# Attention ahead of a mixture of experts: the order of q, k and V loads, the form of two masks, minima per tile, and the place of one copy

## The reference, cut to what matters

```python
batch, n_heads, seq, head_dim = (2, 8, 768, 64);  n_sink, window = (4, 128)
scores = scale * np.matmul(q, k.transpose(0, 1, 3, 2))
keep = is_sink | in_window            # is_sink: key < 4; in_window: 0 <= query - key < 128
scores = np.where(keep, scores, -1000000000.0)
a = np.exp(scores - np.max(scores, axis=-1, keepdims=True))
a = a / (np.sum(a, axis=-1, keepdims=True) + 1e-09)
attn_out = np.matmul(a, v)
```

## Time and profile before

| what | us |
|---|---|
| timed executions | 810.29, 810.45, 813.3; median 810.45 |
| profiled execution | 813.45 |
| its span, first to last instruction | 811.7 |
| PE busy in the span | 768.5 |
| DVE, ACT, POOL busy | 508.9, 285.6, 314.4 |
| first scores / last value matmuls of the attention | 7.0 / 127.7 |

### The profile page before, as it was taken

How to read it: one execution, slowest core, us unless ns; L and a number is a source line. 1 busy time by engine, 2 the same in 40 slices (tenths; PEclk the granted TensorE clock), 3 DMA queues, 4 the chain that set the end, 5 groups by cost and what they waited for, 6 DMA issues and landing times.

```text
span 811.7 us, 13212 instructions
## 1 busy us (share of the span) xinstructions
PE 768.5 (95%) x4198; PEld 631.6 (78%) x4199; DVE 508.9 (63%) x874; ACT 285.6 (35%) x594; POOL 314.4 (39%) x331
## 2 busy tenths in 40 slices
PE   8878794899999999999999999998999999999997
PEld 4666673788888888888888888886888888888886
DVE  5555686444545545445445445457998888888776
ACT  6665571303030300303012300045554555544453
POOL 5367782846473370925618372660111011000000
PEclk9988997799999999999999999999999999999999
DMA  5445565453544270632616272220100110001001
GB/s 162 152 132 147 174 183 195 155 170 117 170 163 135 73 224 26 200 110 90 194 39 224 86 229 73 74 65 0 53 27 26 52 27 27 0 14 40 0 1 52
DMA packets 49485, 82.85 MB, mean 102 GB/s; under 512 B 18080, under 2 KB 22240, under 8 KB 49440
## 3 DMA queue, kind: packets, MB, share of 16 engines
q1 hardware_dynamic: 31440, 33.89, 12.8%
q10 hardware_dynamic: 13600, 33.96, 12.7%
q0 software_dynamic: 4400, 14.42, 6.4%
HBM read 66.01 MB, written 16.25 MB: 101 GB/s over the span
## 4 chain that ended last, share of the span: by engine, by line
PE 84%; DVE 6%; ACT 3%; DMA 3%; issue 3%; SPq 1%; POOL 0%; ACTq 0%; DVEq 0%; POOLq 0%
PE bank L1297 21%; PE bank L1308 21%; PE bank L1369 15%; PE bank L1350 15%; PE bank L1281 3%; DMA k_in<-in_k 2%; PE bank L1202 2%; PE bank L1274 2%; PE bank L1177 2%; ACT probs L657 2%; PE bank L1186 1%; PE bank L1211 1%; DVE bank L834 1%; PE bank L1161 1%; PE bank L1342 0%
## 5 line engine op out<-in xcount | busy, mean ns | idle before, releaser
L562 POOL TENSOR_TENSOR wgt<-stage,wgt 128x1024 f32 (+1 forms) x64 | 151.2, 2401 | 108.9 <-ACT wgt L720 108.9
L1308 PE MATMUL bank<-wgt,hT 128*128 (+1 forms) x744 | 186.1, 399 | 0.0
L1297 PE MATMUL bank<-wgt,xT 128*128 (+1 forms) x744 | 183.9, 396 | 1.5 <-DVE xT L1043 1.5
L1297 PEld LDWEIGHTS bank<-wgt,xT 128*128 128x128 f32 x744 | 138.4, 189 | 29.4 <-DVE xT L1043 1.7
L720 ACT ACTIVATE wgt<-stage 128x1024 f32 (+1 forms) x64 | 61.6, 1045 | 271.3 <-PE bank L1308 261.2
L1308 PEld LDWEIGHTS bank<-wgt,hT 128*128 128x128 f32 x744 | 135.1, 188 | 25.9
L1369 PE MATMUL bank<-wgt,gT 128*128 128x512 f32 x576 | 141.3, 395 | 4.8 <-DVE gT L1104 4.8
L1350 PE MATMUL bank<-x2T,wgt 128*128 128x512 f32 (+1 forms) x588 | 138.2, 385 | 0.9 <-DVE x2T L1081 0.9
L1369 PEld LDWEIGHTS bank<-wgt,gT 128*128 128x128 f32 x576 | 108.5, 190 | 28.6 <-DVE gT L1104 6.1
L1350 PEld LDWEIGHTS bank<-x2T,wgt 128*128 128x128 f32 x588 | 108.7, 188 | 23.0 <-POOL wgt L634 1.1
L1049 DVE TENSOR_SCALAR h<-bank 128x512 f32<-128x512 f32 x62 | 42.9, 691 | 66.7 <-PE bank L1297 66.7
(11 more groups left out here) (166 smaller groups left out, 955.9 us busy)
## 6 DMA issues: line engine op xcount, KB each, us to landing
stage<-in_moe_w ACTq DMA_DIRECT2D x48, 512.0 KB, 3.7
stage<-in_moe_w SPq DMA_DIRECT2D x16, 512.0 KB, 6.0
y_dram<-y_sb SPq DMA_DIRECT2D x31, 256.0 KB, 2.5
stage<-in_moe_w_in ACTq DMA_DIRECT2D x8, 512.0 KB, 4.5
stage<-in_moe_w_out ACTq DMA_DIRECT2D x8, 512.0 KB, 4.1
v_in<-in_v SPq DMA_DIRECT2D x8, 384.0 KB
x_dram<-x_sb SPq DMA_DIRECT2D x16, 192.0 KB, 3.1
out<-o_sb SPq DMA_DIRECT2D x12, 256.0 KB, 2.1
```

Of the source, the lines that this page charges most:

```text
L562: nc.gpsimd.tensor_tensor(cols(parity, 1, u * UNIT, UNIT), stage[:, u, :], cols(parity, 0, u * UNIT, UNIT).bitcast(fp32), ALU.subtract).th ...
L1297: ins = T.matmul(HA[half][:], xT[:, a, c, :], cols(par, b, c * F + half * 512, 512), start=c == 0 and n == 0, stop=c == NC - 1 and n == 2)
L1308: ins = T.matmul(YB[kk % 2][:], hT[:, a, c, :], cols(par, b, NC * UNIT + c * DM, DM), start=c == 0 and n == 0, stop=c == F // P - 1 and n ...
```

## The change

Five edits. SP sends q and k one pair further ahead: those of pair 2 in front of its loop, and in turn i those of pair i + 1, in front of V of pair i, each with a wait for the split of the pair whose buffer they take. The masks with the constant are one `scalar_tensor_tensor` (mask times 1e9 plus the scores) in place of a masked copy, so that the tensor `far` is made only under `window < P`. The minima are taken for each unit right behind its mask. ScalarE takes the exponential of the step's first unit ahead of the copy of the second one's transposed probabilities.

```diff
-    far = route.tensor("far", [P, P], fp32)
+        far = route.tensor("far", [P, P], fp32)
...
+            sp.wait_ge(qk_ready, 4)
+            load_qk(2, 0)
             for i in range(2, NP):
-                sp.wait_ge(qk_ready, 4 * (i - 1))
-                load_qk(i, i % 2)
+                if i + 1 < NP:
+                    sp.wait_ge(qk_ready, 4 * i)
+                    load_qk(i + 1, (i + 1) % 2)
                 sp.wait_ge(pv_ready, QT * (i - 1))
                 load_v(i, i % 2)
                 store_x(i - 2)
...
-            nc.gpsimd.memset(far[:], FAR)
...
             if window < P:
+                nc.gpsimd.memset(far[:], FAR)
...
                 if u > 0:
                     pT_step(u - 2)
+                exp_step(u)
+                if u > 0:
                     pT_step(u - 1)
-                exp_step(u)
                 exp_step(u + 1)
...
                 if t == 0:
-                    V.copy_predicated(own, heads(first_cut[:].bitcast(u32)), heads(far[:])).then_inc(merged, 1)
+                    V.scalar_tensor_tensor(own, heads(first_cut[:]), FAR, own, ALU.mult, ALU.add).then_inc(merged, 1)
...
                 if t == 1:
...
-                    V.copy_predicated(own[:, :, 0:NS], heads(later[:, 0:NS].bitcast(u32)), heads(far[:, 0:NS])).then_inc(merged, 1)
+                    V.scalar_tensor_tensor(own[:, :, 0:NS], heads(later[:, 0:NS]), FAR, own[:, :, 0:NS], ALU.mult, ALU.add).then_inc(merged, 1)
...
-            def row_minima(u, count):
+            def row_minima(u):
...
-                V.tensor_reduce(rt["nb"][:, 2 * b:2 * (b + count)], banks[:, 2 * b:2 * (b + count), SEC:2 * SEC], AX.X,
-                                ALU.min).then_inc(bias_ready, count)
+                V.tensor_reduce(rt["nb"][:, 2 * b:2 * b + 2], SC[b][:, :, SEC:2 * SEC], AX.X, ALU.min).then_inc(bias_ready, 1)
...
                 merge(u)
+                row_minima(u)
+                merge(u + 1)
+                row_minima(u + 1)
                 if u == 0:
-                    row_minima(0, 1)
-                merge(u + 1)
-                if u == 0:
-                    row_minima(1, 1)
                     qk_remainder(0, 2)
                     qk_remainder(0, 3)
-                else:
-                    row_minima(u, 2)
```

## The result

The changed kernel takes 788.8 us in the median of four executions (787.92 to 788.88), the kernel before 810.97 (810.29 to 813.3). The ratio is 0.9719 with a 95% interval of 0.9698 to 0.9741: 22.2 us faster. The profiled execution took 788.75 us, its span is 787.0.

The account below looks back on a forecast made before the run. In attention pairs 2 to 5, late k loads held ScalarE, and TensorE behind it waited and then ran at a slower clock. 20.55 us with 1.3 and 0.3 makes 22.15; 810.45 - 22.15 = 788.3 us, range 784 to 795.

Parts of the forecast that it names:

- The loads: q and k sent a pair of heads sooner end ScalarE's waits and the slow clock: 21.25 us at most, pairs 2-6.
- SP finds the new wait fulfilled: SP's queue: the buffer is already free, so V, stores and weights behind the new wait keep their times.
- not the cause: Rival: something else holds ScalarE at the same place; only 1.6 us would stay, 809 us; chance 0.04.
- slower: Rival: SP stands at the new wait and weight loads come late; some 24 us slower, 834 us; chance 0.03.
- TensorE is the limit: Attention, pair 1: lasts 11.61 us with TensorE busy 11.48 us at clock 1.00, taken as what TensorE needs.
- worth nothing: Minima per unit: first exponential can start 0.7 us sooner, no gain where TensorE is full.
- 11.75 us for each of pairs 2 to 6: Attention: allowed length per pair, since all engines fill the same 11.6 us; 79.30 - 58.75 = 20.55 us gained.
- The first rival: GpSimd or VectorE's split of q and k becomes the bound: pairs of 12.25 to 13.32 us, 791.6 to 797; chance 0.20.
- Pair 7: Last pair of heads: TensorE waits behind the minima; minima per unit take 1.3 us of its 1.7 us excess.
- The masks: VectorE: first tile's mask falls from 797 ns to 0.43 us, freeing 2.9 us; on the path counted within the pairs.
- Exponential ahead of the copy: ScalarE: first unit's result comes at most 0.7 us sooner, usable only in pair 0; 0.3 us taken.
- The sum: Whole change: 20.55 us for pairs 2 to 6, with 1.3 and 0.3, makes 22.15 us.

Follow-up runs that it names:

- loads alone: Only the new order of the q and k loads, on the kernel before: 793.37 us against 814.01, ratio 0.9748.
- weights spread: Changed kernel with the first expert's weights sent earlier and GpSimd's 24 weight steps spread evenly from unit 6 to 45: 785.87 us against 812.31, ratio 0.9674.
- loads and minima: Changed kernel with the old masks and the old order of ScalarE put back: ratio 0.9721 to the kernel before.
- old masks: Changed kernel with the two masked copies of the constant put back: ratio 0.9734 to the kernel before.

## Why the prediction was right, point by point

The forecast was 788.3 us in a range of 784 to 795, faster with a chance of 0.94; 788.8 was measured.

- **The loads** carry it, as said: 20.55 us was taken for pairs 2 to 6 and 20.6 measured for the loads alone. The place (ScalarE ahead of the rounding), the queue and the slow clock behind the waits are shown by the waits that went and by the clock of 1.00 in pairs 2 to 6. "SP finds the new wait fulfilled" is so from the loads of pair 4 on, not for those of pair 3, where it cost nothing; the rivals "not the cause" and "slower" did not occur. That pair 6 needs the masks for its own excess was wrong: it falls from 12.25 to 11.56 us with the loads alone.
- **"TensorE is the limit" at 11.61 us a pair** was mis-sized: 10.96. The 11.48 us of busy time in pair 1 held stops inside the groups of scores that the profile counts as busy (1.34 us for 12 matmuls that take 1.00 after). So "worth nothing" where TensorE is full was too little for the minima per unit: with the loads on time they are worth 0.5 us in pair 2, and with the new order of ScalarE 6 us in all.
- **11.75 us for each of pairs 2 to 6** came out at 11.39 on average, from two errors that offset each other: pairs 2 and 3 lie below the supposed limit, pairs 4 to 6 above the true one by 0.5 to 0.9.
- **The first rival** did occur in pairs 4 to 7, through the split and not through the cuts: VectorE late, no TensorE wait for GpSimd. Its price was too high (pairs of 12.25 to 13.32). Long splits are there from pair 2 on, but in pairs 2 and 3 VectorE is busy 8.57 and 9.63 of 10.96 us and makes up for them.
- **Pair 7** was to give 1.3 us and gave 0.1: the same meeting of engines (a k split of 1.65 us at its start), with VectorE at 12.56 us busy. With the weights spread it falls to 11.64.
- **The masks** at 0.43 us: 0.42 in all eight. On the path they are worth 1.2 us by the ratios, which these runs do not tell from nothing.
- **Exponential ahead of the copy**: the 0.3 us taken for pair 0 came as 0.5, the later pairs gave it back, so about nothing in all, but only with minima per unit; the prediction did not see that the one without the other loses 1 us a pair.
- **The sum** of 22.15 us against 22.2 between the medians is closer than its terms, and that is luck: between the two profiles it is 24.7, with 22.3 in pairs 2 to 6 in place of 20.55 and 0.1 in pair 7 in place of 1.3; 0.5 lies ahead of the scores and 1.4 behind the attention, where the change does nothing.

## What to carry to other kernels

Read the lateness of a load from the queue that sends it: what is ahead of it there, and which wait holds the one in front; moving it ahead by one buffer was worth more here than all arithmetic around it. When a stall goes, the same work runs denser, and the next limit is found where two engines that had been kept apart by the stall now meet: list which of their instructions read SBUF side by side, and spread out the one that can be moved (here 24 weight steps, some 3.7 us by the ratios, where the edits other than the loads gave 2.4). An instruction moved ahead in an in-order queue is only as early as its latest input; move it together with the edit that makes that input early, and try each alone.

## What the runs showed of the hardware

- TensorE's busy time in a profile is not a floor: 11.48 us in one trace, 10.96 in another, for a pair's same matmuls at clock 1.00.
- GpSimd's reads and VectorE's splits hold each other up. A q split takes 527 to 529 ns beside a fill, up to 1310 beside a cast and up to 1573 beside a subtraction; a subtraction of 512 columns takes 1.27 us by itself and up to 1.59 beside splits.
- Cutting a GpSimd subtraction of 512 columns (1.27 us) into four of 128 made them 0.46 us each in the median, and up to 0.79 beside splits: by 1.27 and 0.46, an estimate of 0.2 us for a fixed part.
- The first 18 matmuls of the expert stage took 6.00 us in the kernel before, 4.39 in the changed one and 7.10 with the weights spread, though each waits 1.51 us before them. The granted clock around them was 0.72 (150 to 156 us), 1.00 (126 to 131) and 0.62 (122 to 131). Of all 13 profiles four have 4.37 to 4.41 us there, eight 5.87 to 6.01 and one 7.10, and no edit tells the four from the rest (loads and minima is one of them, old masks is not). What decides between the levels there is not settled; it is up to 2.7 us that no edit here meant to move, 1.6 of it between the two profiles above, and part of the steps between executions may be that.
